# Attention on one core: the bits, the x products, the weighted sum and the turned rows at other steps of a head

## The chip, the cores and the metric

The kernel runs on one core of a Trainium2 chip as one hand-written program with a stream of instructions for each engine: PE (TensorE), DVE (VectorE), ACT (ScalarE), POOL (GpSimd) and SP (SyncE, which here only issues DMAs). The engines meet at semaphores alone. The metric is the device time of one launch in microseconds; the kernel before takes 792.99 us (median of 3 runs, 792.52 to 793.07).

## The reference

Three layers in a row. The change touches only the first, attention with a mask of equal hash buckets; 2 batches of 8 heads, 768 rows of 64:

```python
q_bits = (einsum(q, proj) > 0)            # 6 bits; k_bits in the same way
mask   = q_bucket[:, :, :, None] == k_bucket[:, :, None, :]
scores = scale * (q @ k.T);  scores = where(mask, scores, -1e9)
attn   = softmax(scores);    out = attn @ v
```

Its output is x, 1536 tokens of 512. The second layer routes each token to one of 8 experts (192 tokens each, the highest logit of `x @ w_gate` first) and runs `relu(x @ w1) @ w2`; the third is `silu(x @ w_in) @ w_out`.

## The kernel before

**The tiles.** The 16 heads of both batches run one after the other, in 8 pairs: pair 0 is written out, pairs 1 to 6 are one hardware loop on each engine, pair 7 is written out. Head h has 6 score tiles of 128 query rows by 768 keys, and a head is 6 steps t = 0 to 5, one per tile. Buffers that exist twice (`k_parts`, `q_parts`, `k_bits`, `q_bits`, `probs_t`, `v_quarters`) go by the parity of h. The bank `score_ps` exists once.

**One tile.** PE makes the scores of tile n+2 in step n (4 matmuls, L1240 and L1241) once the minimum of tile n+1 has read the bank. DVE moves them out with the row minimum of the negated scores (`max_tile`, L881), ACT makes the exponentials and row sums (`exp_tile`, L535), DVE transposes them in 32x32 blocks (L959). On DVE the order in a step is the transpose of tile n, then the minimum of tile n+2.

**Work beside the tiles, for other heads.** It goes through two PSUM banks, `work_ps` and `pv_ps`, in turns; a fill on PE waits for the drain before the last one (`s_work_free`).
- rows: k and q of a later head are turned by PE (L1212, two halves each, 3 transposes a half) and drained by ACT to `k_parts` and `q_parts` (`drain_work`, L526). A DMA on SP's queue then copies the high part of k to `k_bits` (`cross`).
- bits: for each half of k and of q two matmuls with the projection (L1214/L1215 and L1218/L1219), drained by ACT as signs (L529). POOL finishes them (`finish_bits`: L742, L759, L762), which the scores of that head wait for.
- weighted sum: for the head before, 96 calls in 24 blocks, 192 records (L1255), split over the steps by `SHARE = [0, 6, 6, 8, 0, 4]` blocks; ACT copies the result out (`turned`, L542).
- x product: the weighted sum times a matrix that turns it and makes the gate's logits (L1225, 12 records); DVE scales it by the inverse row sums (`drain_x`, L869 and L874). POOL adds the logits (L771).
- inverse row sums: DVE adds 1e-9 (L889) and inverts (L890), each followed by a wait for its own end, behind the sixth step of the head (`invert`).
- POOL also splits the loaded rows in high and low parts (`split_rows`, L734 and L736), and in the first head of a pair a piece of the third layer's weights (`split_w_in`, L778 and L780).

**What sets the order.** `events(p, first, last)` gives for each step what goes into the first and the second place; PE, ACT and DVE each walk it. In a head h of the loop: step 0 turns q of h+1 (both halves), step 1 makes the k bits of h+1, step 2 the q bits, step 4 the x product of h-2, step 5 turns k of h+2. The second place stands behind that step's part of the weighted sum. ACT copies out the weighted sum of h-2 at the start of step 0.

**The opening.** Before the loops PE turns the rows of head 0, makes its bits, and makes scores of tiles 0 and 1 with filling matmuls between (`keep_busy`). POOL splits the rows of head 1 and then finishes the bits of head 0.

**The end.** In head 15 PE turns a row of the first batch's best logits (`row_of_first_batch`) at step 1, and behind the last step makes the weighted sum of head 15 in two parts with the x product of head 14 between them.

## Time and profile before

| | |
|---|---|
| median of 3 runs | 792.99 us |
| profiled execution: its own time / its span | 793.57 / 791.8 us |
| busy in the span: PE, DVE, ACT, POOL | 750.3, 478.5, 269.4, 156.3 us |
| attention: first scores to the end of the last x product | 14.09 to 270.98 us |
| 96 score tiles: DVE minimum, ACT exponential, mean of one | 947 ns, 939 ns |
| granted TensorE clock over the span | 0.988 of full speed |

Times in a row count from the start of the span. A PE record's duration has the way through the array in it, so the distance between two starts is what it keeps PE for; where a row shows `[0.67 <-DVE ...]`, the engine stood idle that long and this is what ended it. Routing, experts and the third layer follow at 271 us and are the same in both kernels.

### The profile page before, as it was taken

What the parts mean: (1) busy time and instruction counts of PE and PEld (TensorE: products, weight loads), DVE (VectorE), ACT (ScalarE), POOL (GpSimd) and SP (SyncE); (2) the same over time, 40 slices, a digit from 0 to 9 for tenths busy, and PEclk for the clock granted to TensorE, in tenths of its full rate; (3) what the DMA queues carried; (4) which work ended last, traced back from release to release, by engine and by line L of the source; (5) the groups of instructions that cost most, each with busy time, mean ns of one, the idle gap of its engine ahead of it and who ended that gap; (6) DMA issues with size and microseconds to landing.
All of it is one profiled execution on the core that took longest, in us unless ns stands there. A gap on an engine that the chain in (4) does not pass through costs nothing.

```text
span 791.8 us, 19346 instructions
## 1 busy us (share of the span) xinstructions
PE 750.3 (95%) x7774; PEld 630.6 (80%) x7780; DVE 478.5 (60%) x1097; ACT 269.4 (34%) x551; POOL 156.3 (20%) x193
## 2 busy tenths in 40 slices
PE   7799999999997899999999999999999999999996
PEld 4567777777776658999999999988887888878885
DVE  3778877877877888977977932553233432343321
ACT  3676776776774301222222111321103111120111
POOL 5334436446446010110110100000002000020001
PEclk9899999999999999999999999999999999999999
DMA  6343753654652043633634637700001000010001
GB/s 129 63 98 73 170 125 75 160 123 88 149 119 83 23 142 113 219 133 130 222 138 131 229 134 270 274 16 1 1 0 54 0 0 0 0 53 0 0 0 53
DMA packets 58194, 75.07 MB, mean 95 GB/s; under 512 B 28736, under 2 KB 43072, under 8 KB 57120
## 3 DMA queue, kind: packets, MB, share of 16 engines
q1 hardware_dynamic: 54592, 67.12, 29.4%
q0 software_dynamic: 2208, 7.21, 2.8%
q8 instruction: 36, 0.59, 0.3%
q10 hardware_dynamic: 1344, 0.04, 0.1%
q14 instruction: 14, 0.11, 0.0%
HBM read 64.92 MB, written 6.29 MB: 90 GB/s over the span
## 4 chain that ended last, share of the span: by engine, by line
PE 81%; DVE 7%; issue 6%; ACT 2%; DMA 2%; POOL 1%; DVEq 1%; ACTq 0%; POOLq 0%
PE quad_ps L1530 17%; PE quad_ps L1431 11%; PE quad_ps L1419 10%; PE quad_ps L1255 8%; PE score_ps L1513 8%; PE quad_ps L1513 7%; PE score_ps L1240 4%; PE score_ps L1241 3%; PE work_ps L1361 3%; DVE att_area L881 2%; PE pv_ps L1225 1%; PE work_ps L1225 1%; PE quad_ps L1264 1%; DVE att_area L874 1%; DMA area<-x_rows,ids_now 1%
## 5 line engine op out<-in xcount | busy, mean ns | idle before, releaser
L1530 PE MATMUL quad_ps<-y_s,w_in_s 128*128 128x512 f32 x576 | 137.8, 390 | 2.7 <-DVE y_s L1162 2.0
L1530 PEld LDWEIGHTS quad_ps<-y_s,w_in_s 128*128 128x128 f32 x576 | 107.9, 188 | 26.2 <-DVE y_s L1162 2.8
L1180 DVE TENSOR_TENSOR gate<-quad_ps,sig 128x512 f32<-128x512 f32 x48 | 33.2, 692 | 146.4 <-ACT sig L666 146.4
L881 DVE TENSOR_SCALAR_CACHE_REDUCE att_area<-score_ps 128x768 f32<-128x768 f32 x96 | 90.9, 947 | 49.0 <-PE score_ps L1241 48.7
L535 ACT ACTIVATE att_area<-att_area 128x768 f32<-128x768 f32 x96 | 90.1, 939 | 71.0 <-DVE att_area L881 69.5
L666 ACT ACTIVATE sig<-quad_ps 128x512 f32<-128x512 f32 x48 | 28.7, 598 | 210.5 <-PE quad_ps L1530 210.5
L1419 PE MATMUL quad_ps<-area,experts_w 128*128 128x192 f32 x512 | 96.1, 334 | 1.5 <-ACT area L626 1.2
L1240 PE MATMUL score_ps<-k_parts,q_parts 128*128 128x512 f32 x192 | 73.1, 381 | 19.5 <-DVE att_area L881 12.8
L1431 PE MATMUL quad_ps<-area,experts_w 128*128 128x192 f32 x512 | 87.2, 328 | 0.0
L1419 PEld LDWEIGHTS quad_ps<-area,experts_w 128*128 128x128 f32 x512 | 81.8, 190 | 2.1 <-ACT area L626 2.1
L1431 PEld LDWEIGHTS quad_ps<-area,experts_w 128*128 128x128 f32 x512 | 82.9, 190 | 0.0
L1513 PE MATMUL score_ps<-w_out_s,gate_s 128*128 128x512 f32 x288 | 72.6, 389 | 0.0
L1513 PE MATMUL quad_ps<-w_out_s,gate_s 128*128 128x512 f32 x288 | 72.6, 389 | 0.0
L395 POOL DMA_INDIRECT out<-w_out_raw,ids x12 | 11.9, 995 | 286.7 <-ACT w_out_raw L671 284.0
L1240 PEld LDWEIGHTS score_ps<-k_parts,q_parts 128*128 128x128 f32 x192 | 36.9, 192 | 38.6 <-DVE att_area L881 23.8
L1513 PEld LDWEIGHTS quad_ps<-w_out_s,gate_s 128*128 128x128 f32 x288 | 54.1, 188 | 11.2
L1513 PEld LDWEIGHTS score_ps<-w_out_s,gate_s 128*128 128x128 f32 x288 | 54.0, 188 | 11.2
L1241 PE MATMUL score_ps<-k_bits,q_bits 128*128 128x512 f32 x192 | 62.2, 344 | 0.2 <-issue 0.2
L824 POOL DMA_INDIRECT area<-x_rows,ids_now x16 | 20.1, 1253 | 207.2 <-DVE ids_now L1105 204.8
L630 ACT ACTIVATE area<-quad_ps 128x192 f32<-128x192 f32 x64 | 21.2, 331 | 88.5 <-PE quad_ps L1419 88.5
L959 DVE STREAM_TRANSPOSE att_area<-att_area 128x768 f32<-128x768 f32 x48 | 46.7, 974 | 3.2 <-DVE att_area L890 3.2
L959 DVE STREAM_TRANSPOSE experts_w<-att_area 128x768 f32<-128x768 f32 x48 | 46.7, 973 | 0.3
(202 smaller groups left out, 1100.9 us busy)
## 6 DMA issues: line engine op xcount, KB each, us to landing
experts_w<-in_moe_w SPq DMA_DIRECT2D x16, 2048.0 KB, 9.3
att_area<-in_v SPq DMA_DIRECT2D x64, 192.0 KB, 4.1
experts_w<-in_moe_w_in SPq DMA_DIRECT2D x8, 512.0 KB, 5.6
w_out_raw<-in_moe_w_out SPq DMA_DIRECT2D x4, 1024.0 KB, 9.0
experts_w<-in_k SPq DMA_DIRECT2D x16, 192.0 KB, 3.2
experts_w<-in_q SPq DMA_DIRECT2D x16, 192.0 KB, 3.6
k_bits<-k_parts SPq DMA_DIRECT2D x16, 192.0 KB, 4.7
x_rows<-att_area SPq DMA_DIRECT2D x8, 384.0 KB, 3.6
```

The source lines that it names most:

```text
L535: nc.scalar.activation(probs[c % 3], probs[c % 3], ACT.Exp, scale=-1.0, bias=neg_max[:, c:c + 1], accum_out=row_sum[:, c:c + 1]).then_inc( ...
L666: nc.scalar.activation(sig[:, :], layer_ps[f % 2][:, 0:GT], ACT.Sigmoid).then_inc(s_sig, 1)
L881: nc.vector.tensor_scalar(probs[c % 3], score_ps[0][:, 0:S], 0.5 * BIG, None, ALU.min, ALU.min, accum_out=neg_max[:, c:c + 1]).then_inc(s_ ...
L959: nc.vector.transpose(probs_t[p][:, t, :], probs[c % 3]).then_inc(s_pt, 1)
L1180: nc.vector.tensor_tensor(gate[:, :], layer_ps[f % 2][:, 0:GT], sig[:, :], ALU.mult).then_inc(s_mul, 1)
L1240: nc.tensor.matmul(score_ps[0][:, cols], q_parts[p][:, tile], k_parts[p][:, cols], start=True, stop=False)
L1241: done = nc.tensor.matmul(score_ps[0][:, cols], q_bits[p][:, tile], k_bits[p][:, cols], start=False, stop=True)
L1255: done = nc.tensor.matmul(quad_ps[side, 512 * a:512 * a + QT], v_quarters[p][rows, b % 4, D * (b // 4):D * (b // 4 + 1)], probs_t[p][rows, ...
L1419: done = nc.tensor.matmul(layer_ps[j % 2][:, 0:CAP], w1_cols[r % 2][:, c, j, :], xg_t[:, c, :], start=(c == 0), stop=(c == DC - 1))
L1431: done = nc.tensor.matmul(layer_ps[c % 2][:, 0:CAP], w2_sb[r % 2][:, j, c * P:(c + 1) * P], h_t[:, j, :], start=(j == 0), stop=(j == F1C - 1))
L1513: done = nc.tensor.matmul(out_ps[m], gate_s[:, fo % RING_S, a, m * P:(m + 1) * P], w_out_s[:, fo, b, :], start=(fo == 0 and a + b == 0), s ...
L1530: done = nc.tensor.matmul(layer_ps[f % 2][:, 0:GT], w_in_s[:, a, w_cols], y_s[:, c, b, :], start=(c == 0 and a + b == 0), stop=(c == DC - ...
```

## The change

`events` now gives a list for each step. In a head h of the loop: step 0 has k bits, k bits, q bits of h+1; step 1 the last q bits and the x product of h-2; steps 2 and 3 each half of the weighted sum of h-1; step 4 turns k of h+2, step 5 turns q of h+2, two halves each. ACT drains in that order, with the tile's exponential behind the first drain of a step, and copies the weighted sum out at step 4 of the same head. DVE adds 1e-9 to the row sums behind the first transpose of the next head and inverts behind the second one, without a wait for its own end, and drains x at step 2. In the opening POOL finishes head 0's bits before it splits head 1's rows, and PE turns all rows of head 1 behind the scores of tile 1. In the last head the row of best logits moves to step 4, and the weighted sum of head 15 is one run behind the x product of head 14. SP's waits are renumbered (`k_drained`), and its queue keeps its order. No arithmetic is changed.

```diff
-            opening = first and p == 0
-            kinds = [] if last and p else PREP_KINDS if opening else PREP_KINDS[2:]
-            e = {(i // 2, i % 2): (kind, i % 2, i, 1) for i, kind in enumerate(kinds)}
-            if not first:
-                e[(4, 0)] = ("x", 0, len(e), 2)
-            if not last:
-                for half in range(2):
-                    e[(5, half)] = ("k", half, len(e), 2)
+            bits = [] if last and p else [("k_bits", 0, 1), ("k_bits", 1, 1), ("q_bits", 0, 1), ("q_bits", 1, 1)]
+            x = [] if first else [("x", 0, 0)]
+            rows = [] if last else [("k", 0, 2), ("k", 1, 2), ("q", 0, 2), ("q", 1, 2)]
+            at_t = {0: bits[0:3], 1: bits[3:4] + x, 4: rows[0:2], 5: rows[2:4]}
```

ACT, in the opening and in one step:

```diff
-            exp_tile(0, 0)
-            exp_tile(1, 1)
+            for t in range(2):
+                exp_tile(t, t)
+                for half in range(2):
+                    i = PREP + 2 * t + half
+                    drain_work("q" if t else "k", half, i, 1, work_banks[i % 2])
...
-                        if t == 0 and not first:
-                            act.wait_ge(s_work_full, w)
-                            turned(2 * g + p - 2)
+                        if t == 4 and not (first and p == 0):
+                            if not first:
+                                act.wait_ge(s_work_full, w)
+                            turned(2 * g + p - 1)
+                        for slot, (kind, half_, i, ahead) in enumerate(ev[t]):
+                            if slot == 1:
+                                next_exp(n, c, last)
                             if kind != "x":
                                 drain_work(kind, half_, w, (p + ahead) % 2, bank_of(first, p, i))
                             w = w + 1
```

POOL, in the opening and in the last head:

```diff
+            finish_first_bits()
             split_rows(1, 1, 0)
-            finish_first_bits()
...
                     if last and p == 1:
-                        for i in (PAIRS - 2, PAIRS - 1):
-                            split_beside(i, h)
-                    if (4, 0) in ev:
+                        split_beside(PAIRS - 2, h)
+                    if not first:
                         add_logits(h - 2)
+                    if last and p == 1:
+                        split_beside(PAIRS - 1, h)
```

DVE, in one step:

```diff
+                        if t == 0 and not (first and p == 0):
+                            add_to_sums(h - 1, 1 - p)
+                        if t == 1 and not (first and p == 0):
+                            invert(h - 1, 1 - p)
                         if not (last and c + 2 >= 2 * T):
                             max_tile(n + 2, (c + 2) % (2 * T))
```

PE, in the opening, in one step and at the end:

```diff
-            keep_busy(3, idle_bank)
+            for i in range(4):
+                w = PREP + i
+                fill_work(PREP_KINDS[i], i % 2, max(PREP, w - 1), 1, 1, work_banks[w % 2])
...
-            SHARE = [0, 6, 6, 8, 0, 4]
+            SHARE = [0, 0, 12, 12, 0, 0]
...
+                        for kind, half, i, ahead in ev[t]:
                             if kind == "x":
                                 fill_work(kind, half, u - 1, h - 2, p, bank_of(first, p, i))
...
-            weighted(HEADS - 1, 1, 0, 8, PAIRS - 1)
-            fill_work("x", 0, None, HEADS - 2, 0, work_banks[0], x_free=HEADS - 3)
-            weighted(HEADS - 1, 1, 8, KB - 8, PAIRS - 1)
-            fill_work("x", 0, None, HEADS - 1, 1, work_banks[1], x_free=HEADS - 2)
+            pe.wait_ge(s_row, 2)
+            fill_work("x", 0, None, HEADS - 2, 0, work_banks[0], x_free=HEADS - 2)
+            weighted(HEADS - 1, 1, 0, KB, PAIRS - 1)
+            fill_work("x", 0, None, HEADS - 1, 1, work_banks[1], x_free=HEADS - 1)
```

PE in the loop, before: step 4 of a first head, from behind its scores (L1225 is the x product, L1240 and L1241 are scores, L1212 turned rows, L1255 the weighted sum).

```order
L1200 REGISTER_ALU
L1225 ISA
L1225 MATMUL work_ps<-att_area 128x72 x6
L1237 REGISTER_ALU
L1240 MATMUL score_ps<-k_parts,q_parts 128x512
L1241 MATMUL score_ps<-k_bits,q_bits 128x512
L1240 MATMUL score_ps<-k_parts,q_parts 128x256
L1241 MATMUL score_ps<-k_bits,q_bits 128x256
L1209 ISA
L1212 MATMUL pv_ps<-ident,experts_w 128x128 x3
L1255 MATMUL quad_ps<-experts_w,att_area 64x192 x16
L1212 MATMUL work_ps<-ident,experts_w 128x128 x3
```

PE now, step 1 and the start of step 2 (L1234 is the x product, L1249 and L1250 are scores, L1264 the weighted sum). The x product has moved in front of the whole weighted sum, behind the bits:

```order
L1209 REGISTER_ALU
L1232 ISA
L1234 ISA
L1234 MATMUL work_ps<-att_area 128x72 x6
L1246 REGISTER_ALU
L1249 MATMUL score_ps<-k_parts,q_parts 128x512
L1250 MATMUL score_ps<-k_bits,q_bits 128x512
L1249 MATMUL score_ps<-k_parts,q_parts 128x256
L1250 MATMUL score_ps<-k_bits,q_bits 128x256
L1257 ISA
L1258 ISA
L1264 MATMUL quad_ps<-experts_w,att_area 64x192 x48
```

Each run of the weighted sum is now 48 calls long instead of 16 to 32, and only score matmuls stand between the two runs.

ACT in the loop, before, from the second q rows on (L529 drains bits, L535 is the exponential):

```order
L523 REGISTER_ALU
L529 ACTIVATE k_bits<-work_ps,below 64x384
L534 REGISTER_ALU
L535 ACTIVATE att_area<-att_area 128x768
L523 REGISTER_ALU
L529 ACTIVATE k_bits<-pv_ps,below 64x384
L523 REGISTER_ALU
L529 ACTIVATE q_bits<-work_ps,below 64x384
L534 REGISTER_ALU
L535 ACTIVATE att_area<-att_area 128x768
L523 REGISTER_ALU
L529 ACTIVATE q_bits<-pv_ps,below 64x384
```

ACT now, from the start of the loop (L531 drains bits, L537 is the exponential):

```order
L531 ACTIVATE k_bits<-work_ps,below 64x384
L536 ISA
L537 ACTIVATE att_area<-att_area 128x768
L525 REGISTER_ALU
L531 ACTIVATE k_bits<-pv_ps,below 64x384
L525 REGISTER_ALU
L531 ACTIVATE q_bits<-work_ps,below 64x384
L525 REGISTER_ALU
L531 ACTIVATE q_bits<-pv_ps,below 64x384
L536 REGISTER_ALU
L537 ACTIVATE att_area<-att_area 128x768
```

Three drains of bits stand in a row behind the second exponential, where one exponential stood between each two pairs.

DVE at the end of the loop, before (L881 is the minimum, L889 and L890 are the sum and the inverse, L984 closes the loop):

```order
L959 STREAM_TRANSPOSE experts_w<-att_area 128x768
L878 REGISTER_ALU
L881 TENSOR_SCALAR att_area<-score_ps 128x768
L886 ISA
L889 TENSOR_SCALAR att_area<-att_area 128x6
L347 ISA
L890 RECIPROCAL att_area<-att_area 128x6
L347 REGISTER_ALU
L984 REGISTER_ALU
L984 COMPARE_AND_BRANCH
```

DVE now, the same place in the middle of the loop (L970 is the transpose, L885 the minimum, L895 and L901 the sum and the inverse):

```order
L885 TENSOR_SCALAR att_area<-score_ps 128x768
L970 STREAM_TRANSPOSE experts_w<-att_area 128x768
L890 ISA
L895 TENSOR_SCALAR att_area<-att_area 128x6
L882 REGISTER_ALU
L885 TENSOR_SCALAR att_area<-score_ps 128x768
L970 STREAM_TRANSPOSE experts_w<-att_area 128x768
L899 ISA
L901 RECIPROCAL att_area<-att_area 128x6
```

The sum and the inverse stand behind transposes of the next head; the last work in front of the loop's end is now a minimum.

## Rows read from the trace of the kernel before

**Rows 1.** Timeline, PE, one head: start us, us, engine line op, count [idle before <-releaser].

```profile
136.50 1.45 PE L1225 MATMUL pv_ps<-att_area 128*128 x12
137.75 0.48 PE L1240 MATMUL score_ps<-k_parts,q_parts 128*128 128x512 f32 x1
...
138.55 0.49 PE L1212 MATMUL work_ps<-ident,experts_w 128*128 128x128 f32 x3
...
143.11 0.50 PE L1240 MATMUL score_ps<-k_parts,q_parts 128*128 128x512 f32 x1 [0.67 <-DVE att_area L881]
...
144.35 1.23 PE L1255 MATMUL quad_ps<-experts_w,att_area 32*64 32x192 f32 x48
...
149.52 1.56 PE L1255 MATMUL quad_ps<-experts_w,att_area 32*64 32x192 f32 x64
```

**Rows 2.** Timeline, DVE, one head pair and the last pair.

```profile
140.32 0.17 DVE L889 TENSOR_SCALAR att_area<-att_area 128x6 f32<-128x6 f32 x1
...
141.22 0.98 DVE L959 STREAM_TRANSPOSE att_area<-att_area 128x768 f32<-128x768 f32 x1 [0.51 <-DVE att_area L890]
...
144.11 0.96 DVE L881 TENSOR_SCALAR_CACHE_REDUCE att_area<-score_ps 128x768 f32<-128x768 f32 x1 [0.17 <-PE score_ps L1241]
...
170.48 0.17 DVE L889 TENSOR_SCALAR att_area<-att_area 128x6 f32<-128x6 f32 x1
...
246.02 2.13 DVE L889 TENSOR_SCALAR att_area<-att_area 128x6 f32<-128x6 f32 x1
```

**Rows 3.** Timeline, ACT, one head and the opening.

```profile
25.95 0.58 ACT L529 ACTIVATE k_bits<-pv_ps,below 64x384 fp32r<-64x384 f32 x1
26.43 0.56 ACT L529 ACTIVATE q_bits<-work_ps,below 64x384 fp32r<-64x384 f32 x1
...
143.09 0.94 ACT L535 ACTIVATE att_area<-att_area 128x768 f32<-128x768 f32 x1 [0.17 <-DVE att_area L881]
...
144.03 0.47 ACT L526 ACTIVATE q_parts<-pv_ps 128x384 fp32r<-128x384 f32 x1
144.52 0.58 ACT L529 ACTIVATE k_bits<-work_ps,below 64x384 fp32r<-64x384 f32 x1
145.13 0.94 ACT L535 ACTIVATE att_area<-att_area 128x768 f32<-128x768 f32 x1
...
146.18 0.58 ACT L529 ACTIVATE k_bits<-pv_ps,below 64x384 fp32r<-64x384 f32 x1
```

**Rows 4.** Timeline, PE, DVE and POOL in the opening.

```profile
9.13 0.55 DVE L847 TENSOR_SCALAR k_bits<-quad_ps 64x384 fp32r<-64x384 f32 x1
...
12.98 0.91 POOL L748 TENSOR_SCALAR k_bits<-k_bits,k_shift 64x768 fp32r<-64x768 f32 x1
...
14.09 0.47 PE L1240 MATMUL score_ps<-k_parts,q_parts 128*128 128x512 f32 x1 [2.50 <-POOLq L751]
...
30.02 0.77 PE L1240 MATMUL score_ps<-k_parts,q_parts 128*128 128x512 f32 x1 [2.82 <-POOL q_bits L762]
...
35.41 0.75 PE L1240 MATMUL score_ps<-k_parts,q_parts 128*128 128x512 f32 x1
```

**Rows 5.** Timeline, PE, the last two heads.

```profile
246.16 0.50 PE L1240 MATMUL score_ps<-k_parts,q_parts 128*128 128x512 f32 x1 [1.01 <-DVE att_area L881]
...
250.30 0.50 PE L1240 MATMUL score_ps<-k_parts,q_parts 128*128 128x512 f32 x1 [3.17 <-DVE att_area L881]
...
269.45 1.53 PE L1225 MATMUL pv_ps<-att_area 128*128 128x72 f32 x12 [1.06 <-ACT att_area L542]
```

**Rows 6.** Timeline, POOL, one head and the last pair.

```profile
144.66 0.82 POOL L742 CAST q_bits<-q_parts 64x768 fp32r<-64x768 f32 x1 [4.93 <-ACT q_parts L526]
...
245.75 2.37 POOL L780 TENSOR_TENSOR w_in_s<-experts_w,w_in_s 128x1024 fp32r<-128x1024 f32 x1
```

**Rows 7.** Stretches, PE: us, busy (count), granted clock, DMA share, GB/s.

```profile
30.00:32.00 2.00, 1.62 (x4) 0.50 0.36 81
246.00:248.00 2.00, 0.97 (x4) 1.00 0.64 177
```

More of the change, by code:

```diff
@@ L587, in _ @@
             pair(PAIRS - 1, False, True)
-            act.wait_ge(s_work_full, W_LAST)
-            turned(HEADS - 2)
             act.wait_ge(s_const, 3)
@@ L791, in pair @@
                     h = 2 * g + p
-                    ev = events(p, first, last)
                     if not (last and p == 1):
-                        finish_bits(h + 1, 1 - p, PREP + 4 if first and p == 0 else preps_of(h + 1) + 2)
+                        finish_bits(h + 1, 1 - p, k_drained(h + 1) + 2)
                     if not last:
@@ L965, in pair @@
                             best_of_first_batch()
[L966 to L980 removed]
+                        if t == 2 and not first:
+                            if p == 0:
+                                dve.wait_ge(s_xw, 16 * g)
+                            dve.wait_ge(s_logits, h - 1)
+                            dve.wait_ge(s_norm_step, 2 * (h - 1))
+                            i = len(ev[0]) + len(ev[1]) - 1
+                            drain_x(w + i, p, bank_of(first, p, i))
+                    w = w + sum(len(ev[t]) for t in range(T))
             pair(0, True, False)
@@ L1303, in pair @@
                         if not (last and c + 2 >= 2 * T):
-                            scores((c + 2) % (2 * T), h + 1 if t >= T - 2 else h, u, n + 2, g + (p if t >= T - 2 else 0))
-                        if (t, 0) in ev:
-                            if last and p == 1:
-                                pe.wait_ge(s_row, 2)
-                            kind, half, i, ahead = ev[(t, 0)]
+                            scores((c + 2) % (2 * T), h + 1 if t >= T - 2 else h, n + 2, g + (p if t >= T - 2 else 0))
+                        for kind, half, i, ahead in ev[t]:
                             if kind == "x":
@@ L1311, in pair @@
                             else:
-                                fill_work(kind, half, u if kind == "k" and not first else u - 1, h + ahead, (p + ahead) % 2, bank_of(first, p, i))
+                                fill_work(kind, half, u if kind == "k" and half == 0 and not first else u - 1, h + ahead,
+                                          (p + ahead) % 2, bank_of(first, p, i),
+                                          x_free=h if kind == "k" and half == 1 and not first else None)
                                 u = u + 1
-                        if last and p == 1 and t == 1:
+                        if last and p == 1 and t == T - 2:
                             row_of_first_batch(u)
@@ L1317, in pair @@
                             weighted(h - 1, 1 - p, sum(SHARE[0:t]), SHARE[t], g if p else g - 1)
-                        if (t, 1) in ev:
-                            kind, half, i, ahead = ev[(t, 1)]
-                            fill_work(kind, half, u - 1, h + ahead, (p + ahead) % 2, bank_of(first, p, i),
-                                      x_free=h - 1 if kind == "k" and not first else None)
-                            u = u + 1
             pair(0, True, False)
```

94 lines of the change are left out of this document (43 added, 51 removed).

## The prediction

> **What bounds the kernel now.** I read the stretches of the span first. PE is busy for 750.3 of 791.8 us, DVE and ACT for much less, so the first question is whether PE is full or waits in small pieces. The chain of waits answers it: over the loop it runs through PE, and leaves it only where DVE's minimum holds the one score bank. Then I read the timelines of PE, DVE, ACT and POOL over one pair of heads side by side, and last the two ends of attention, where PE stands idle longest. Routing and what follows is the same code in both kernels; I let it only shift.
>
> The pace: from one sum of row sums to the same one a pair later it is 170.48 - 140.32 = 30.16 us, 15.08 a head [rows 2]. In that head PE idles 0.67 us in front of a score tile, waiting for the minimum [rows 1]. A round scores, minimum, scores can't be shorter than 1.00 (scores from 143.11 to the minimum's start at 144.11) + 0.96 + 0.06 = 2.02 us [rows 1, 2]. So a step with less than 2.02 us of PE work is bound by that round, and one with more by PE. Before, each step was filled to about 2 us or more. The new order makes steps 0, 4 and 5 thin and steps 2 and 3 thick, so the question is which chain closes the head.
>
> **The loop, part by part.** I count from M, the end of the minimum of tile 1 of a head, which releases the exponential of tile 1 on ACT (step 5), and go round to the next M.
>
> ACT first. In its new order come the exponential of tile 1, the drain of the second q rows, k bits, the exponential of tile 2, k bits, q bits. From start to start [rows 3]: exponential to copy 144.03 - 143.09 = 0.94; copy to sign 0.49; sign to exponential 145.13 - 144.52 = 0.61; exponential to sign 1.05; sign to sign 26.43 - 25.95 = 0.48; and the last sign takes 0.58. With 0.05 in front and behind that is 4.25 us from M to the moment at which the x product may start, because its PSUM bank is the one that these q bits held. The exponential of tile 2 fits in: its minimum ends 0.05 + 1.00 + 0.96 = 2.01 us behind M, and ACT comes to it at 0.05 + 0.94 + 0.49 + 0.61 = 2.09. PE needs far less for the same work, so it waits for drains here, which it did not before.
>
> Then PE without a gap: x product 137.75 - 136.50 = 1.25; scores of tile 4 138.55 - 137.75 = 0.80 [rows 1]; half of the weighted sum; scores of tile 5, 0.80; the other half. A half is 96 records: 48 take 1.23 and 64 take 1.56 [rows 1], so 0.0206 each, and 1.56 + 32 x 0.0206 = 2.22, 2.24 with the change of tile shape. Sum 1.25 + 0.80 + 2.24 + 0.80 + 2.24 = 7.33. The runs it replaces (two of 48 records, one of 64, one of 32) come to more together, as each pays its start again; that gain is in the sum already.
>
> Last, steps 4 and 5 of the next round, where only the rows are turned beside the scores: two bare rounds, 2 x 1.96 + 0.06 = 3.98.
>
> Round: 4.25 + 7.33 + 3.98 = 15.56. In the x product's case I add 0.09, because after a wait it starts 0.14 behind its release (269.45, the copy having ended at 269.31) instead of 0.05 [rows 5]. So 15.65 a head, against 15.08: **0.57 us a head more**, although PE has less to do. The bounds of this: with every ACT distance as short as possible (exponential to sign 0.94, no late start) 15.45; with the loop's end of DVE exposed (below) 15.86.
>
> *The sum and the inverse on DVE.* Before, they and the loop's end stand in the chain: 141.22 - 140.32 = 0.90 us between the sum and the next transpose, 0.51 of it idle behind a wait for the inverse's own end [rows 2]. Now a minimum of 0.96 us stands in front of the loop's end, and the branch can run beside it. I take it as hidden. The Trainium skill, "Advanced Engine Details and Errata", section "Sequencer Loop", says that other engine instructions can be read and queued while the sequencer executes control; by that rule the branch is hidden, and the trace neither proves nor denies it, as the wait stood in front of it. If it is not hidden, the minimum of tile 2 comes 0.5 later, ACT reaches it 0.42 later, once a pair.
>
> *POOL.* In the middle of attention its instructions keep their lengths. The copy of q's high part follows the second q drain by 0.16 (144.66, the drain of 144.03 having ended at 144.50) [rows 3, 6], the bits of a head are finished 5 us before its scores, rows are split before they are turned at step 4. SP's queue keeps its order; the copy of k's high part has over 10 us, and v and the loads more. I cost all of it at nothing; the margin of each is more than 2 us.
>
> **The opening.** Before, the first scores start at 14.09 behind POOL's L748 (12.98 + 0.91 = 13.89) [rows 4]. Now POOL can begin when DVE's second k bits are out, 9.13 + 0.55 = 9.68: 9.84 + 0.92 for the copy + 0.91 = 11.67, first scores at 11.87. Then scores of tile 1 at 13.87; the rows of head 1 behind them, held by ACT, which drains two before and two behind the exponential of tile 1; scores of tile 2 of head 0 at about 16.6, tile 3 at 19.3 and tile 4 at 21.2 (bits), then bare rounds: 23.2, 25.2, 27.2, and tile 2 of head 1 at 29.2. Before it started at 35.41, behind a wait of 2.82 for POOL's q bits and in a stretch with the granted clock at 0.50, the lower of the two levels [rows 4, 7]. The scores of head 1 begin at 25.2; POOL's constants, now behind the split of head 1's rows, and the bits of head 1 I take as done by then. **Gain 6.2 us**; if those bits are late, what they are late comes off it, as the 2.82 did before.
>
> **Through the heads.** Head 1 has no x product: 15.65 - 1.25 = 14.4. Then 13 heads of 15.65. Tile 2 of head 15 starts at 29.2 + 14.4 + 203.5 = 247.1, before at 246.16 [rows 5]: the opening's gain is spent, with 0.9 more.
>
> **The end.** Before, from 246.16 to the end of the last x product, 269.45 + 1.53 = 270.98, it takes 24.8 us [rows 5]. In it PE is idle for 3.17, as the sum on DVE took 2.13 instead of 0.17 us: it ended at 248.15, when POOL's L780 (245.75 + 2.37 = 248.12) did [rows 2, 6]. Now POOL's piece of weights for head 14 is done before that sum, and the next waits for the inverse of head 14, so the collision goes. New: a round 2.0; scores 0.8; x 1.25; scores 0.8; 2.24; scores 0.8; 2.24; the copy out and two row copies on ACT with the row's turning beside them, 1.7; x 1.3; the weighted sum of 192 records 1.56 + 128 x 0.0206 = 4.2; copy and release 1.0; x 1.5: together 20.0. **Gain 4.8 us.** DVE's comparisons stay beside the weighted sum as before.
>
> So the last x product ends at 267.1 instead of 270.98, -3.9, if PE's clock stays at its upper level, 2.4 GHz. But heads 14 and 15 now have four rounds in a row with scores alone (steps 4, 5, 0, 1), and head 0 two to three. The clock stood at 0.50 after idle times of 2.82 and 3.17 us; a stretch of two us with 0.97 busy kept 1.00, but was short [rows 4, 5, 7]. Eight us half idle are not shown here. I take one fall to 1.2 GHz near the end. Its price from the fall before: two rounds from 30.02 to 35.41, 5.39 instead of 4.04, so 1.4 [rows 4]; a piece of the weighted sum in it makes 1.5.
>
> **Sum.** +0.9 at tile 2 of head 15 (-6.2 of the opening, -0.7 of head 1, 13 x 0.57 = +7.4, and +0.4 as before reached it 0.4 sooner than 35.41 + 14 x 15.08), -4.8 at the end, +1.5 for the clock: -2.4. The profiled execution took 793.57 and lies 0.58 above the median of the runs, so 791.1 there, and **790.6** for the median.
>
> **Rivals.**
> - *The clock never falls* (0.20): -3.9, 789.1. For it: no idle time over 1.1 us is left in attention. Against it: the thin rounds are many in a row.
> - *The loop's end on DVE is exposed* (0.18): 7 x 0.42 = 2.9 more, 793.5. For it: the 0.51 of row 141.22. Against it: no wait for an own end is left there.
> - *ACT's chain is shorter* (0.08): 0.2 less a head, 788.0.
> - *The clock falls at both ends* (0.06): 1.4 more, 792.0.
> - *The sum meets POOL's copy* (0.08), the one on the slow side. The sum stands 0.82 behind M (the minimum frees DVE 0.08 before M, a transpose keeps it 0.90); POOL's copy starts at 0.05 + 0.94 + 0.47 + 0.16 = 1.62 and lasts 0.82 [rows 6]. If in the heads behind the loop's end DVE comes more than 0.80 late, the sum is held to 2.44, the minimum of tile 2 starts at 2.6 instead of 1.1, and the head is 1.5 longer: 7 x 1.5 = 10.5, 801. The point that decides is whether the sum starts before 1.62. That such a hold exists the 2.13 us of 246.02 show. The Trainium skill, "SBUF — State Buffer", section "Who interferes with whom", says that a `tensor_scalar` in a two-port mode and a GpSimd instruction take a shared pair of ports for the whole instruction, and the later one blocks. By that rule, the trace agrees, and the price stands only if DVE comes second; at 0.80 of margin it speaks for no loss.
>
> **How the numbers follow.** The forecast has 0.40, with a range of its own of 789.3 to 792.6 (13 heads at plus or minus 0.12, the clock's 1.5). From no change a measurement can tell 0.2%, 1.6 us: 791.4 to 794.6 is "same". Faster: 0.26 of the forecast, 0.19 and 0.08 of the two fast rivals, 0.04 of the rest, 0.57. Same: 0.14 + 0.13 + 0.04 = 0.31. Slower: 0.04 of the exposed loop and 0.08 of the collision, 0.12. The range 787.8 to 795.0 leaves out the collision and the tails.
>
> **What would show it.** Heads of 15.6 to 15.7 us in the loop, without a difference between the first and the second head of a pair; ACT with three bit drains in a row and x starting right behind the third; PE idle in steps 0, 4 and 5; first scores near 11.9, tile 2 of head 1 near 29; the sum always 0.17 us; last x product ending near 267 to 269. I am wrong if heads take 15.1 or less (then PE, not the drains, closes the head), or if the granted clock is at 0.50 for more than one stretch.

## The result, and the profile after

The changed kernel takes 798.3 us (median of 18 runs, 793.05 to 801.99); the kernel before 793.5 beside it (18 runs, 790.9 to 796.96). The ratio is 1.0056, 95% interval 1.0038 to 1.0074: 0.6% slower, where 790.6, 0.3% faster, was forecast. Its profiled execution took 797.15 (span 795.4).

| profiled execution | before | predicted | after |
|---|---|---|---|
| first scores | 14.09 | 11.87 | 11.67 |
| tile 2 of head 1 starts | 35.41 | 29.2 | 29.27 |
| a head in the loop | 15.08 | 15.65 | 15.83 |
| tile 2 of head 15 starts | 246.16 | 247.1 | 249.43 |
| from there to the end of the last x product | 24.8 | 20.0 + 1.5 | 24.77 |
| last x product ends | 270.98 | 268.6 | 274.20 |

The opening came as forecast [rows 4], in the timeline of PE after:

```profile
11.67 0.47 PE L1249 MATMUL score_ps<-k_parts,q_parts 128*128 128x512 f32 x1 [0.28 <-POOLq L756]
...
29.27 0.50 PE L1249 MATMUL score_ps<-k_parts,q_parts 128*128 128x512 f32 x1
```

One head in the loop, PE after [rows 1]. Columns as there: start, duration, engine, line, operation, count, idle time in front and its releaser.

```profile
142.62 0.44 PE L1227 MATMUL pv_ps<-q_parts,proj_high 128*128 128x384 f32 x1 [0.39 <-ACT k_bits L531]
...
143.33 1.55 PE L1234 MATMUL work_ps<-att_area 128*128 x12
144.69 0.48 PE L1249 MATMUL score_ps<-k_parts,q_parts 128*128 128x512 f32 x1
...
145.56 2.21 PE L1264 MATMUL quad_ps<-experts_w,att_area 32*64 32x192 f32 x96
147.70 0.50 PE L1249 MATMUL score_ps<-k_parts,q_parts 128*128 128x512 f32 x1
...
148.59 2.21 PE L1264 MATMUL quad_ps<-experts_w,att_area 32*64 32x192 f32 x96
150.73 0.50 PE L1249 MATMUL score_ps<-k_parts,q_parts 128*128 128x512 f32 x1
...
152.75 0.50 PE L1249 MATMUL score_ps<-k_parts,q_parts 128*128 128x512 f32 x1 [0.41 <-DVE att_area L885]
```

PE waits 0.39 in front of the last bits, and the x product starts 0.30 behind the end of the drain of its bank (142.47 + 0.56 below). This delay is 0.30 in the first head of a pair and 0.20 in the second; in head 14, which is written out and not in the loop, it is 0.05 (237.99, the drain having ended at 237.94). What takes the time in the loop isn't shown. Then PE works without a gap and idles 0.41 in front of the scores of 152.75, in a thin round. In the same head ACT has the three bit drains in a row [rows 3]; the x product needs the second of them:

```profile
139.80 0.47 ACT L528 ACTIVATE q_parts<-pv_ps 128x384 fp32r<-128x384 f32 x1
...
140.94 0.94 ACT L537 ACTIVATE att_area<-att_area 128x768 f32<-128x768 f32 x1
...
141.99 0.57 ACT L531 ACTIVATE k_bits<-pv_ps,below 64x384 fp32r<-64x384 f32 x1
142.47 0.56 ACT L531 ACTIVATE q_bits<-work_ps,below 64x384 fp32r<-64x384 f32 x1
143.28 0.58 ACT L531 ACTIVATE q_bits<-pv_ps,below 64x384 fp32r<-64x384 f32 x1 [0.24 <-PE pv_ps L1228]
```

DVE after [rows 2]: the transpose at 138.75 starts the moment the minimum of 137.86 leaves the engine, across the loop's end, and the sum takes 0.13 in every head. Six heads, 60.58 to 155.54, are 94.96 us: 15.83 each. They alternate: the second head of a pair takes 15.75, the first 15.86 to 15.95.

```profile
60.58 0.13 DVE L895 TENSOR_SCALAR att_area<-att_area 128x6 f32<-128x6 f32 x1
...
138.75 0.97 DVE L970 STREAM_TRANSPOSE att_area<-att_area 128x768 f32<-128x768 f32 x1
139.64 0.13 DVE L895 TENSOR_SCALAR att_area<-att_area 128x6 f32<-128x6 f32 x1
...
155.54 0.13 DVE L895 TENSOR_SCALAR att_area<-att_area 128x6 f32<-128x6 f32 x1
```

The end is where the profile has something that the forecast had only in small. Stretches of 2 us: busy time and count of PE, PEld, DVE, ACT and POOL, then the granted clock, DMA share and GB/s [rows 7]:

```profile
246.00:248.00 2.00, 0.94 (x6) 0.65 (x5) 1.62 (x3) 1.06 (x2) 0.00 (x0) 1.00 0.68 184
248.00:250.00 2.00, 0.94 (x5) 0.65 (x4) 1.83 (x4) 1.01 (x3) 0.00 (x0) 0.98 1.10 227
250.00:252.00 2.00, 0.94 (x4) 0.60 (x3) 1.60 (x6) 0.72 (x3) 0.00 (x0) 0.50 0.86 251
252.00:254.00 2.00, 2.00 (x9) 1.81 (x9) 1.33 (x3) 0.74 (x2) 0.99 (x1) 0.50 0.01 2
...
258.00:260.00 2.00, 2.00 (x64) 1.71 (x56) 1.69 (x5) 1.03 (x2) 1.22 (x2) 0.50 0.00 0
260.00:262.00 2.00, 2.00 (x54) 1.45 (x50) 0.27 (x1) 0.00 (x0) 1.92 (x2) 0.96 0.68 205
```

PE is busy 0.94 of each 2 us in the thin rounds, never idle for more than 1.06 at a time, and from about 250 to 260 the clock is at 0.50, the lower of its two levels (1.2 GHz). In that time stand not only thin rounds, where a slow PE costs little, but the x product of head 13 and half a weighted sum, 3.65 instead of 2.21 us:

```profile
249.43 0.50 PE L1249 MATMUL score_ps<-k_parts,q_parts 128*128 128x512 f32 x1 [1.06 <-DVE att_area L885]
...
253.18 2.67 PE L1234 MATMUL pv_ps<-att_area 128*128 128x72 f32 x12
...
257.15 3.65 PE L1264 MATMUL quad_ps<-att_area 32*64 32x192 f32 x96
...
265.63 1.56 PE L1234 MATMUL work_ps<-att_area 128*128 128x72 f32 x12 [1.00 <-ACT experts_w L562]
267.11 4.55 PE L1264 MATMUL quad_ps<-experts_w,att_area 32*64 32x192 f32 x192
...
272.67 1.53 PE L1234 MATMUL pv_ps<-att_area 128*128 128x72 f32 x12 [1.01 <-ACT att_area L544]
```

The other executions have a time and a mean clock only, and the two go together. Of the 18, the fastest had a mean granted clock of 0.996 (793.05 us), the profiled one 0.990 (797.15), the slowest 0.982 (801.99); a straight line through all has 6.0 us for each 0.01 and leaves 0.7 us of scatter.

### The profile page after: what moved, and what is told of

The parts are those of the page before. It is cut to its first block, busy times and chain, and to the rows that moved or that the text cites. A ratio compares the mean times of both kernels' runs of the same rounds, so it can differ in the third digit from the quotient of the medians.

```text
span 795.4 us, 19347 instructions
## 1 busy us (share of the span) xinstructions
PE 753.1 (95%) x7772; PEld 634.3 (80%) x7777; DVE 475.0 (60%) x1097; ACT 270.5 (34%) x551; POOL 155.9 (20%) x193
## 4 chain that ended last, share of the span: by engine, by line
PE 80%; issue 8%; ACT 4%; DVE 4%; DMA 2%; POOL 1%; DVEq 0%; ACTq 0%; SPq 0%; POOLq 0%
PE quad_ps L1535 17%; PE quad_ps L1424 10%; PE quad_ps L1436 10%; PE quad_ps L1264 9%; PE score_ps L1518 8%; PE quad_ps L1518 7%; PE score_ps L1249 5%; PE score_ps L1250 3%; PE work_ps L1366 2%; ACT k_bits L531 2%; PE pv_ps L1234 2%; PE work_ps L1234 2%; DMA area<-x_rows,ids_now 1%; PE quad_ps L1273 1%; ACT att_area L537 1%
## 5 line engine op out<-in xcount | busy, mean ns | idle before, releaser
L885 DVE TENSOR_SCALAR_CACHE_REDUCE att_area<-score_ps 128x768 f32<-128x768 f32 x96 | 91.9, 958 | 64.7 <-PE score_ps L1250 63.4
L537 ACT ACTIVATE att_area<-att_area 128x768 f32<-128x768 f32 x96 | 90.0, 938 | 75.1 <-DVE att_area L885 74.2
L1249 PE MATMUL score_ps<-k_parts,q_parts 128*128 128x512 f32 x192 | 73.7, 384 | 12.7 <-DVE att_area L885 11.6
L1249 PEld LDWEIGHTS score_ps<-k_parts,q_parts 128*128 128x128 f32 x192 | 36.5, 190 | 34.4 <-DVE att_area L885 20.0
L1250 PE MATMUL score_ps<-k_bits,q_bits 128*128 128x512 f32 x192 | 61.4, 342 | 0.0
L970 DVE STREAM_TRANSPOSE experts_w<-att_area 128x768 f32<-128x768 f32 x48 | 46.7, 973 | 0.2 <-ACT att_area L537 0.2
L970 DVE STREAM_TRANSPOSE att_area<-att_area 128x768 f32<-128x768 f32 x48 | 46.7, 972 | 0.0
```

Source lines behind the costliest of these rows:

```text
L537: nc.scalar.activation(probs[c % 3], probs[c % 3], ACT.Exp, scale=-1.0, bias=neg_max[:, c:c + 1], accum_out=row_sum[:, c:c + 1]).then_inc( ...
L885: nc.vector.tensor_scalar(probs[c % 3], score_ps[0][:, 0:S], 0.5 * BIG, None, ALU.min, ALU.min, accum_out=neg_max[:, c:c + 1]).then_inc(s_ ...
L970: nc.vector.transpose(probs_t[p][:, t, :], probs[c % 3]).then_inc(s_pt, 1)
L1249: nc.tensor.matmul(score_ps[0][:, cols], q_parts[p][:, tile], k_parts[p][:, cols], start=True, stop=False)
L1250: done = nc.tensor.matmul(score_ps[0][:, cols], q_bits[p][:, tile], k_bits[p][:, cols], start=False, stop=True)
```

## The experiments

Medians, ranges, and ratios to the kernel before with 95% intervals; two versions whose intervals overlap can't be told apart by them. The mean granted clock is that over all runs of a kernel; it was 0.9885 for the changed kernel and 0.988 for the one before.

| run | what it is | us | ratio | clock |
|---|---|---|---|---|
| e1 | changed kernel, thin rounds at the end filled | 793.8 (793.0 to 796.2) | 0.9999 (0.9986 to 1.0012) | 0.994 |
| e2 | before + opening | 790.3 (788.7 to 792.0) | 0.9948 (0.9929 to 0.9967) | 0.987 |
| e3 | e2 + POOL's last piece moved | 793.1 (790.6 to 795.5) | 0.9989 (0.9974 to 1.0005) | 0.983 |
| e4 | changed kernel, one more sign on ACT | 802.2 (800.6 to 804.4) | 1.0096 (1.0075 to 1.0117) | 0.990 |
| e5 | e2 + POOL's piece of head 14 moved | 787.7 (785.6 to 789.8) | 0.9934 (0.9914 to 0.9955) | 0.990 |
| e6 | e5 + thin rounds filled | 782.8 (782.0 to 785.5) | 0.9879 (0.9860 to 0.9898) | 0.997 |
| e7 | e2 + sum and inverse moved | 782.3 (781.1 to 787.5) | 0.9875 (0.9848 to 0.9902) | 0.990 |
| e8 | e6 and e7 together | 781.5 (778.5 to 784.5) | 0.9844 (0.9818 to 0.9871) | 0.994 |
| e9 | e7 + weighted sum in two runs | 811.2 (806.4 to 812.5) | 1.0208 (1.0178 to 1.0237) | 0.979 |
| e10 | changed kernel, weighted sum in three runs | 802.9 (800.1 to 806.4) | 1.0112 (1.0086 to 1.0139) | 0.990 |
| e11 | e1 + thin rounds of the opening filled | 794.6 (793.2 to 796.6) | 1.0013 (1.0001 to 1.0025) | 0.995 |
| e12 | e5 and e7 together | 782.0 (780.7 to 783.5) | 0.9852 (0.9830 to 0.9874) | 0.991 |

**e1, is it the thin rounds that let the clock fall?** In PE's loop over the steps, behind `weighted`:

```
+                        if last and (p, t) in [(0, 4), (0, 5), (1, 0), (1, 1)]:
+                            pe.wait_ge(s_x_free, HEADS - 2)
+                            keep_busy(5, work_ps, 320)
```

> The changed kernel, with five bf16 products of a constant (128x320 each, into a PSUM bank that is free there) behind the work of each of the last four thin rounds (steps 4 and 5 of head 14, steps 0 and 1 of head 15). Theory A, the clock fell there because PE was half idle in four rounds in a row: the granted clock stays 1.00 from 248 to 262, the x product of head 13 takes about 1.5 instead of 2.67 us, the half of the weighted sum 2.2 instead of 3.65, the last x product ends near 270 instead of 274.2, and the median falls from 798.3 by about 4 to 794 to 795, with a smaller spread. Theory B, the fall has another cause (what the DMAs or the other engines do at that moment): the clock falls as before and the median stays at 798, or is 0.5 to 1 higher for the added products.

Theory A, with the median a little under its range. The same stretches now have 1.64 and 1.67 of PE busy and keep the clock, with the DMA traffic beside them as high as before:

```profile
248.00:250.00 2.00, 1.64 (x10) 1.06 (x10) 1.83 (x4) 1.01 (x3) 0.00 (x0) 1.00 1.07 225
250.00:252.00 2.00, 1.67 (x9) 1.08 (x9) 1.88 (x5) 1.01 (x2) 0.00 (x0) 1.00 1.04 271
```

And PE's timeline of the end (x product of head 13, added products of a constant, half a weighted sum, the weighted sum of head 15, last x product):

```profile
252.83 1.45 PE L1234 MATMUL pv_ps<-att_area 128*128 128x72 f32 x12
254.12 0.85 PE L1273 MATMUL work_ps<-ones 128*128 128x320 bf16 x5
254.70 0.51 PE L1249 MATMUL score_ps<-k_parts,q_parts 128*128 128x512 f32 x1
...
255.59 2.21 PE L1264 MATMUL quad_ps<-att_area 32*64 32x192 f32 x96
...
264.11 4.16 PE L1264 MATMUL quad_ps<-experts_w,att_area 32*64 32x192 f32 x192
...
269.33 1.53 PE L1234 MATMUL pv_ps<-att_area 128*128 128x72 f32 x12 [1.06 <-ACT att_area L544]
```

From tile 2 of head 15 (250.00) to the end of the last x product it now takes 20.86 us instead of 24.77. The median falls by 4.5 and the range from 9 us to 3. The fall itself cost more than the difference of 3.91, because the last group of added products stands behind an x product, where PE had no idle time, and takes 0.58 (254.12 to 254.70). From tile 2 to the second half of the weighted sum it is 12.19 us in the changed kernel (249.43 to 261.62) against 8.62 here (250.00 to 258.62), or 8.04 without those products: the fall cost 4.15, not 1.5. The other 0.34 are in the last weighted sum, 4.55 instead of 4.16 us at a granted clock of 1.00 in both, and stay unexplained.

**e4, is it ACT's chain that closes the head?** In ACT's `drain_work`:

```
+                    if kind == "q_bits" and half == 0:
+                        nc.scalar.activation(spare[D:P, :], bank[D:P, 0:256], ACT.Sign, scale=-LIFT, bias=below[D:P, :])
```

> The changed kernel with one more ACT instruction a head (a sign over 64x256, whose result nothing reads) right in front of the drain of the first q bits, which releases the bank of the x product. It keeps ACT 0.32 to 0.48 us. Theory A, the head is closed by ACT's drains in front of the x product: each head grows by all of it, 15.80 to 16.1 to 16.3, and the time by 4.5 to 7 us, to 803 to 805. Theory B, PE closes the head and the drains have room: heads stay within 0.1 of 15.80 and the time within 1 us of 798.3.

```profile
162.08 0.46 ACT L533 ACTIVATE spare<-pv_ps,below 64x256 bf16<-64x256 f32 x1
162.44 0.57 ACT L534 ACTIVATE q_bits<-pv_ps,below 64x384 fp32r<-64x384 f32 x1
...
62.04 0.13 DVE L898 TENSOR_SCALAR att_area<-att_area 128x6 f32<-128x6 f32 x1
...
159.29 0.13 DVE L898 TENSOR_SCALAR att_area<-att_area 128x6 f32<-128x6 f32 x1
```

Theory A in the heads: the added sign keeps ACT 0.36 us (162.08 to 162.44), and six heads take 97.25, 16.21 each: 0.38 more. Over 13 heads that is 5 us; the median rose 3.9, less than the 4.5 to 7 expected, at a mean clock a little better than the changed kernel's.

**e2, the opening alone.** POOL's `finish_first_bits` in front of `split_rows(1, 1, 0)`, the opening's events shortened to the bits, and head 1's rows ahead of the loop:

```
-            kinds = [] if last and p else PREP_KINDS if opening else PREP_KINDS[2:]
+            kinds = [] if last and p else PREP_KINDS[4:] if opening else PREP_KINDS[2:]
...
             scores(1, 0, PREP, 1, 0)
-            keep_busy(3, idle_bank)
+            for i in range(4):
+                w = PREP + i
+                fill_work(PREP_KINDS[i], i % 2, max(PREP, w - 1), 1, 1, work_banks[w % 2])
```

> The kernel before with one part of the change alone: the opening (POOL makes the first bits before it splits head 1's rows, and the rows of head 1 are turned ahead of the loop, their drains on ACT behind the first two exponentials). Theory A: this part gives what was predicted of it, 6.2 us, and the loop and the end of the kernel before are untouched: median 793.5 - 6.2 = 787.3. Theory B, the opening's gain is given back later, because the clock then falls elsewhere or head 1 waits for its bits: 790 or more.

Theory B, barely (790 or more): 3.3 gained (before beside it: 793.6), where theory A had 6.2. In its profiled execution the clock is low in the opening, where it wasn't in the changed kernel's, and again at the end:

```profile
24.00:28.00 4.00, 2.84 (x8) 1.89 (x7) 2.27 (x4) 1.61 (x4) 3.31 (x5) 0.50 0.46 104
28.00:32.00 4.00, 2.96 (x11) 2.58 (x12) 3.09 (x7) 1.66 (x4) 0.08 (x1) 0.50 0.00 0
32.00:36.00 4.00, 3.85 (x32) 3.09 (x40) 3.37 (x6) 3.11 (x8) 0.00 (x0) 0.78 0.23 49
...
248.00:252.00 4.00, 4.00 (x58) 3.25 (x56) 2.24 (x4) 1.95 (x5) 3.56 (x3) 0.50 0.13 46
```

Tile 2 of head 15 starts at 243.31 here, 2.85 before 246.16 [rows 5]. In the profiled execution of e3, whose code is the same up to there, it starts at 240.93, with a shorter stretch at 0.50 (24 to 32): 2.4 us between two executions of the same code, in which nothing but the clock is seen to differ.

**e3 and e5, the hold of 2.13 us [rows 2, 6].** e3 moves the last piece of weights behind the addition of head 13's logits. e5, in head 14, moves POOL's `split_beside(beside, h)` in front of `add_logits(h - 2)`.

> As the kernel with the opening alone, and with POOL's order at the end: the logits of head 13 are added between the two last pieces of weights, so that the second piece no longer runs beside DVE's sum of row sums. Theory A: the 2.13 us of that sum fall to 0.2 and the 3.17 us of idle PE with them, and the clock's fall behind them goes too: 2 to 3.5 us less than the opening alone, 784 to 785.3. Theory B: the sum or the tile behind it then waits for something else, for example the rows of best values, which wait for the same pieces of weights: within 0.5 us of the opening alone.

> The opening-alone kernel, and in head 14 POOL's piece of weights in front of the addition of logits instead of behind it, where it ended 2 us too late and held DVE's sum of row sums for 2.13 us. (The previous try moved the wrong piece and left the hold as it was.) Theory A: the sum takes 0.2 us, the idle of PE in front of the scores of head 15 falls from 3.17 to about 1.0, the last x product ends 2.0 us sooner, and the fall of the clock behind that idle goes or not: median 790.3 - 2.0 = 788.3, or 786.8 without the fall. Theory B, the clock falls in the thin rounds there all the same and longer, as in the changed kernel: 789.5 or more.

e3 met neither theory; it moved the wrong piece. The held sum stays as it was (idle of PE 3.16), and the moved piece now holds DVE later, beside the comparisons:

```profile
258.18 2.35 POOL L783 TENSOR_TENSOR w_in_s<-experts_w,w_in_s 128x1024 fp32r<-128x1024 f32 x1
...
258.38 2.21 DVE L907 TENSOR_TENSOR choice<-logits,best 128x48 f32<-128x48 f32 x1
```

DVE's L907 takes 2.21 instead of 0.21 us and ends when POOL's L783 does. That delays the comparisons, the logits of head 14 and ACT behind them, so that the last x product waits 2.00 instead of 1.06. That is about 1 us of e3's loss of 2.9 against e2; the rest goes with its lower clock (0.983 against 0.987). In e5 the sum takes 0.17, the idle in front of the scores of head 15 is 1.21, the clock stays at 1.00 there, and from tile 2 of head 15 to the end of the last x product it takes 21.26 us instead of e2's 25.44. Theory A, with a gain in the median (2.6) between its two values; the two intervals of the runs overlap, so the trace carries this more than the median does. It also says what the end of the change is worth: with hold and fall gone the old end takes 21.26, only 1.0 more than the new one with a full clock (e1's 20.86 without its 0.58).

**e6 and e11, the thin rounds of the opening too.** Both have fillings at the end (e6 four products behind step 5 of head 14 and step 0 of head 15, e11 those of e1) and add them in the opening:

```
+                        if first and p == 0 and t in (2, 3, 4):
+                            keep_busy(4, idle_bank, 320)
```

(e6; e11 has five behind steps 2 and 3 and three behind 4 and 5.)

> As the kernel with the opening and without the hold, and with four products of a constant (128x320, bf16) behind the work of the thin rounds: steps 2, 3 and 4 of head 0, step 5 of head 14, step 0 of head 15. Theory A, thin rounds are what lets the clock fall, in the opening too (where these kernels stand at 0.50 for 6 to 12 us between 24 and 34 us): the granted clock stays 1.00 there, the mean clock of the runs rises from 0.987 to over 0.992, and the median is 3 to 4 us below the kernel without the products. Theory B, the falls in the opening have another cause: within 1 us of it.

> The changed kernel with products of a constant in the thin rounds of both ends: those of the first try (steps 4 and 5 of head 14, steps 0 and 1 of head 15), and five behind steps 2 and 3 and three behind steps 4 and 5 of head 0. That try stood at 793.8 with a fall of 4 us between 24 and 28 us in its profiled execution and a mean clock of 0.994. Theory A, the fall in the opening has the same cause: mean clock 0.996 or more, median 792 to 792.8. Theory B, the opening of this kernel loses nothing to the clock in most executions: within 0.5 of 793.8.

e6: theory A, and more than expected. The clock of the profiled execution is 1.00 all through attention and routing, its mean over the runs 0.997, and the median 4.9 below e5.

e11 met neither theory: it lies 0.9 above e1, outside the 0.5 of B, and the two intervals overlap, so no gain is shown. In the profiled executions the products in the opening did what they should: the clock is 1.00 there, where e1's was low from 24 to 28 us, and the sum of head 1 comes at 44.67 instead of 45.12 (44.56 in the changed kernel), the last x product 0.76 sooner. It is lost again behind the last x product: the DMA that gathers rows for the experts (`area<-x_rows`) takes 5.86 us instead of 5.28, and what follows it 1.1 more. In the same way e6's profiled execution is 1.8 us ahead of e5's at tile 2 of head 15 (e5's clock was low from 26 to 34), takes as long to the last x product, and wins 2.0 more behind it: 0.9 in the routing, where e5's clock is low from 268 to 272 and e6's is not, 0.6 in that DMA (5.15 instead of 5.71), 0.5 later. So half of what e6 gains in these two executions lies in stretches that the products don't touch, and why e6 gains so much more than e11 isn't settled.

**e7 and e9, the loop of the kernel before with one part of the change each.** e7 moves DVE's sum and inverse as the change does (`add_to_sums` behind the first transpose, `invert` behind the second). e9 adds to it:

```
-            SHARE = [0, 6, 6, 8, 0, 4]
+            SHARE = [0, 0, 12, 12, 0, 0]
```

> The opening-alone kernel, and in the loop the part of the change on DVE alone: the sum of row sums behind the first transpose of the next head and the inverse behind the second one, with the loop of the kernel before kept in everything else. Heads of the kernel before take 15.32 and 14.84 us in turn. Theory A: the long one is long because the loop's end and the inverse's own end stand in front of the next transpose; it falls to 14.9, and the median by 7 x 0.45 = 3.1, to 787.1. Theory B: what DVE saves at the head's end it pays in steps 0 and 1, as the minimum of tile 2 comes later behind the sum: heads 15.0 to 15.1, median 790. Theory C: the sum now meets a copy on POOL and is held 0.8 or more a head: 795 or more.

> The kernel with the opening and with the sum and inverse moved on DVE (heads of 14.70 us, PE without idle time), and of the change's loop one part alone: the weighted sum in two runs of 96 records in steps 2 and 3, in place of 48, 48, 64 and 32 records. Bits, rows and x product stay spread over the steps as before. Theory A, thin steps cost because their two-us round can't be filled: steps 0, 1 and 5 fall back on the round of 2.02 us, and a head takes 2.02 + 2.02 + 3.9 + 3.0 + 2.2 + 2.02 = 15.2 us, the median 782.3 + 7 = 789. Theory B, the two runs cost nothing, only the placing of bits and x product does: heads 14.6 to 14.8, median 782.

e7, one pair of heads from sum to sum:

```profile
103.64:118.34 14.70, 14.40 (x250) 11.25 (x249) 11.82 (x24) 10.69 (x22) 6.67 (x9) 1.00 0.76 169
118.34:133.03 14.69, 14.40 (x250) 11.24 (x249) 11.93 (x23) 10.69 (x22) 8.65 (x10) 1.00 0.34 81
```

Heads of 14.70 and 14.69 us, with PE busy 14.40 in both. Theory A, and more than twice its size: not only the long head of a pair became shorter, the short one of 14.84 did too. The median falls 7.9 below e2. In the profiled executions the 13 heads are 5.3 us shorter (191.63 against 196.90); the rest goes with the clock and with a shorter hold at the end; 1.9 of it is won ahead of the loop, where e2's clock was low. Theory C shows in traces: the sum takes 0.33 to 0.37 in every second head, held by 0.2 us, and 1.22 once, in head 14.

e9: theory A in kind, but dearer than its 15.2 a head and 789. The thin rounds make it 15.69 a head (46.21 to 93.29, three heads), 1.0 more than e7. PE waits for minima and for ACT's drains in the thin steps. From the third pair on, where POOL has a piece of weights in each, a second thing comes on top. First the timelines of POOL and DVE:

```profile
161.57 2.36 POOL L783 TENSOR_TENSOR w_in_s<-experts_w,w_in_s  x1 [0.18 <-POOL w_in_s L781]
...
161.73 2.24 DVE L893 TENSOR_SCALAR att_area<-att_area 128x6 f32<-128x6 f32 x1
...
180.22 0.13 DVE L893 TENSOR_SCALAR att_area<-att_area 128x6 f32<-128x6 f32 x1
```

Then the stretches behind it, columns as above:

```profile
162.00:164.00 2.00, 0.81 (x6) 0.33 (x4) 2.00 (x2) 1.43 (x3) 1.93 (x1) 1.00 0.30 67
164.00:166.00 2.00, 1.12 (x6) 0.98 (x6) 1.90 (x5) 1.14 (x3) 0.00 (x0) 0.94 0.23 49
166.00:168.00 2.00, 2.00 (x7) 1.40 (x6) 1.75 (x3) 1.74 (x4) 0.82 (x1) 0.50 0.00 0
```

The sum at the start of a second head of a pair is held until POOL's piece of weights ends (161.57 + 2.36 = 163.93), and that head takes 180.22 - 161.73 = 18.49 instead of 15.7; behind the idle time PE's clock falls to 0.50. The Trainium skill, "SBUF — State Buffer", section "Who interferes with whom", has this: a DVE instruction in a two-port mode and a GpSimd one take the shared ports for a whole instruction, and the later one blocks. The trace agrees, and the price is not the 2.1 us of hold but 2.8 with the fall of the clock in it, every second head.

**e10, does it matter how the weighted sum is cut behind the x product?** `SHARE = [0, 8, 8, 8, 0, 0]` in the changed kernel.

> The changed kernel with its weighted sum in three runs of 64 records behind the x product, in steps 1, 2 and 3, in place of two of 96 in steps 2 and 3. Theory A, the head is a chain (ACT's drains, x product, weighted sum, two thin rounds), in which it doesn't matter how the weighted sum is cut: heads 15.8 to 15.95, one more start of a run, the median 798 to 800. Theory B, it is the two thick steps beside the thin ones that cost: heads 15.5 or less, the median 794 or less.

```profile
146.36 1.55 PE L1234 MATMUL work_ps<-att_area 128*128 x12
147.84 1.56 PE L1264 MATMUL quad_ps<-experts_w,att_area 32*64 32x192 f32 x64
...
150.22 1.56 PE L1264 MATMUL quad_ps<-experts_w,att_area 32*64 32x192 f32 x64
```

Against B, and dearer than A: 16.17 a head (61.86 to 158.90), 0.34 more. The three runs take 3 x 1.49 = 4.47 instead of 2 x 2.14 = 4.28, and the x product with a run behind it 1.48 instead of 1.36: 0.31 of the 0.34. The head is a chain, and every start of a run in it counts. The median of 802.9 is above the 798 to 800 of A.

**e8 and e12, the versions that beat both.**

> All of these together: the opening, no hold in head 14, the sum and inverse moved on DVE, the products of a constant in the thin rounds. If the gains add, each at its theory A: 790.3 - 2.0 - 3.1 - 3.0 = about 782. If a shorter loop brings the clock down, or the parts stand in one another's place: 785 to 788.

> The kernel with the opening and the moved sum and inverse, and POOL's piece of weights in head 14 in front of the addition of logits; no products of a constant. The sum of head 14 takes 1.22 us there without this edit, behind that piece. Theory A: it falls to 0.13 and the time by 1.1, to 781.2. Theory B: nothing, because POOL's next pieces move later by as much and are waited for: 782.3.

e8 has the lowest median, 781.5, 1.6% below the kernel before, but its interval overlaps those of e7 and e12. Expected were 782; it is not the sum of its parts, since e7 has most of it alone. e12: the sum of head 14 takes 0.13, and the median is 0.4 below e7's, which these runs can't tell from nothing; its theories stay undecided. In the profiled execution of e12 the clock fell all the same at 238 us, behind two idle times of 1.01 and 1.06, and stood at 0.50 from 238 to 240. Left in e7, e8 and e12 are also stretches at 0.50 in the routing (between 264 and 272), which the kernel before has too (between 278 and 282).

## Why the prediction was wrong, point by point

- *The opening: right* (29.27 against 29.2). The profiled execution was lucky there: in those of e1, e4 and e10, which share this opening, the clock is low between 24 and 30 us, and the sum of head 0 comes at 30.61, 31.26 and 31.12 instead of 30.03. The opening's worth in the runs is smaller too, 3.3 in e2, whose profiled execution has such a fall.
- *What closes a head: right in mechanism, too small.* The chain is ACT's drains, x product, scores, weighted sum, two thin rounds, as e4 shows by its 0.38 for 0.36. Its terms were off: the x product starts 0.30 or 0.20 behind its drain, not 0.14, and this drain is the second of the three in a row, not the third, as the signs to look for had it; it keeps PE 1.36, not 1.25; scores keep it 0.87 to 0.89 in front of the weighted sum, not 0.80; the halves 2.14, not 2.24. In the head of the rows above: from the end of the minimum (137.86 + 0.96 = 138.82) 4.51 to the x product, 7.40 to 150.73, 3.99 to 154.72, together 15.90; the mean of six heads is 15.83, 0.18 over the forecast. From 29.27 to 249.43 it took 220.2 where 217.9 were predicted: 2.3 of the 5.6 us that the last x product is late.
- *"I take one fall to 1.2 GHz near the end. Its price [...] makes 1.5": the step that failed.* The fall came where it was feared, but lasted 10 us, and x product, scores and half a weighted sum lay in it. It cost 4.15 (above, against e1), 2.65 too little in the forecast. The price had been read from a fall in which only thin rounds stood. The end without it took 24.77 - 4.15 = 20.62 and not 20.0: 0.34 of this are the unexplained ones in the last weighted sum, and the terms as they are written add up to 19.8. Together 3.3 of the 5.6.
- *The routing and the median.* Behind the last x product 0.4 more than before in the profiled execution; and the profiled execution lies 1.15 below the median, not at it, as it had a better clock (0.990) than the mean (0.9885); by the 6.0 us for each 0.01 that is 0.9 of the 1.15. 5.6 + 0.4 + 1.15 + 0.58 (which the forecast had taken off for the median of before) = 7.7, the whole miss.
- *The loop's end on DVE is hidden: right* (138.75 above). "Without a difference between the first and the second head" isn't: the first is 0.11 to 0.20 longer, 0.10 of it the later start of its x product.
- *The sum meets POOL's copy: did not happen* in the changed kernel, 0.13 in every head; the mechanism exists and cost 2.8 a pair in e9, though with another instruction of POOL, its piece of weights.
- *What wasn't asked:* what each part is worth in the other order. The moved sum and inverse are worth 7.9 with the loop of before (e7), 5.3 of it in the heads; in the changed kernel's, where ACT's chain closes the head, that gain doesn't show (this is argued: the changed kernel without them wasn't run). From e7 (782.3) to the changed kernel (798.3) the rest of the change, above all the order of bits, x product and weighted sum, costs 16: 15.83 - 14.70 = 1.13 in 13 heads, 14.7, and the rest of it in the ends and the clock. The two runs alone bring 1.0 a head in e9.

## What to carry to other kernels

Where a round of three engines has a shortest length (here 2.02 us), spread the work of the fullest engine evenly over the rounds: what a thick step adds a thin one doesn't give back, since no round gets shorter than that, and thin ones in a row can let TensorE's clock fall. Price a fall by what stands behind it, not by the idle time that lets it in; where thin rounds can't be avoided, products of a constant in them are cheap to try. And before a change is judged as a whole, run its parts: here one part was worth 1%, and the rest of the change took it and more.

## What the runs showed of the hardware that was not expected

- The clock fell with PE idle for no more than 1.06 us at a time, busy 0.94 of each 2 us, and stayed at 0.50 to about 260, though PE was busy the full 2 us from 252 on. The Trainium skill, "TensorE: Matmul & The Clock Gate", section "A second HAM failure mode: psum-queue depth-cycling", tells of a kernel whose clock swings between its levels because TensorE idles briefly and often between groups of products; the trace agrees, and e1, in which these idle times are shorter (0.36) and the clock stays, bears it out. By the falls before, behind idle times of 2.82 and 3.17 us [rows 4, 5], a forecast would have seen none here.
- How much it falls varies between executions of the same code: 0.982 to 0.996 in mean for one kernel, with 9 us between their times. A single profiled execution doesn't tell whether a kernel has this cost.
- Whether POOL holds an instruction of DVE hangs on small shifts of the order: the same sum of head 14 took 0.13 (e12), 1.22 (e7) and 2.13 us [rows 2].
